# Linear attention and Fourier-mixing MLP: the output products of the chunk pairs regrouped by row mode, under a new order of all engines

## The chip, the cores and the metric

The kernel runs on one core of a Trainium2 chip. The metric is device time in microseconds (us) of one execution. Before the change three runs gave 195.79, 196.08 and 197.27 us, so a median of 196.08 us. The engines are TensorE (PE; its weight loads are PEld), VectorE (DVE), ScalarE (ACT), GpSimd (POOL) and SyncE (SP, which here issues the loads and stores).

## The reference

The inputs are r, k, v, w of shape (4 batches, 8 heads, 768 steps, 48), u of (8, 48), and the weights w_ch1 (384 x 1536) and w_ch2 (1536 x 384). Cut to what matters:

```python
# linear attention with a decaying state, per batch and head
for t in range(S):
    cur = einsum('bhd,bhe->bhde', u * k[t], v[t])
    y[t] = einsum('bhd,bhde->bhe', r[t], state + cur)
    state = w[t][..., None] * state + einsum('bhd,bhe->bhde', k[t], v[t])
# then, with x = y laid out as (4, 768, 384)
mixed = real(fft(fft(x, axis=1), axis=2))
u = x + mixed
un = (u - mean(u)) / sqrt(var(u) + 1e-6)
out = u + maximum(un @ w_ch1, 0) @ w_ch2
```

## The kernel before, in words

**Tiling.** Each batch's 768 steps are cut in six chunks of 128. A chunk's decays become exponentials of running sums (matmuls at L755 and L759, in the first batch L615 and L616), r and k are scaled by them (`rkh`), transposed, and multiplied into a 128 x 128 score block per head (`amat`, L681 or L825), which VectorE masks into `ah` (L687 or L838). The output of a chunk is a masked product of `ah` with v plus r times the state before the chunk.

**The first batch goes in chunk pairs** (`pair`, from L592). Two chunks are loaded interleaved, so that a chunk's rows lie in one half of the 128 partitions, once for even steps and once for odd ones. Its products therefore use 64 of TensorE's 128 rows. In `ymat` (L719 to L731) a chunk's output takes: two half-row matmuls with the bonus term (L721, 384 columns each), and then for each of four head pairs one full-row matmul with the state (L725, 96 columns; not for the first chunk, which has no state yet) and four half-row matmuls with `ah` (L729, 48 columns each). All add up in one PSUM bank. There are six such outputs, five of them with the state. `state` (L701 to L711) is likewise one full-row matmul (L703) and eight half-row ones (L707). The other three batches go chunk by chunk (`attention`), where only `amat` (L825) uses fewer than 128 rows.

**After a batch's attention** its output is folded (`fold`: sums and differences, `xf`), mixed by two rounds of matmuls (L944, L945, L947; then L970), normalised, transposed, and sent through the two MLP products (W1 at L1017, W2 at L1035). W1 and W2 are loaded by one transfer each, issued on GpSimd's queue (L586).

**Order.** The kernel records every operation with the tiles that it reads and writes, and then places them by two tables that were computed in advance: `ORDER` lists each engine's operations by number, `BANKS` lists which PSUM bank holds which tile when. Engines run their list strictly in order and wait on semaphores for what an operation needs from another engine. The times that stand in the `op(...)` calls served the planner that made the tables; they do not enter the emitted program. Where VectorE, ScalarE or GpSimd may do an operation, the table also decides which one does.

**Filler.** `early` issues NE matmuls on a constant tile (L1055) at the start, and NW further operations of the same kind (`warm`, L1072 and L1073) stand in the table between real work. Their results are not used. All operations that only move data through `vec`, `evict` and the like show the helper's line (L450, L473, L474), so they are told apart by their tiles.

Of the kernel before, what the change touches and what calls it, by code (L numbers as in the profile page):

```python
# [20 lines left out]
NE = 13  # L21

NW = 5
# [37 lines left out]
    "act": (  # L61
# [12 lines left out]
    "dve": (  # L74
# [71 lines left out]
class _Prog:  # L146
# [17 lines left out]
    def op(self, eng, dur, fn, r=(), w=(), sem=None, xfer=0, port=(), tiled=False):  # L164


        if not isinstance(dur, dict):
            dur = {eng: dur}
# [156 lines left out]
def bass_rwkv6_finch__then__fnet_fourier_mix_kernel(  # L325
# [11 lines left out]
    DM = H * D  # L337
# [86 lines left out]
    def ps(t):  # L424
        return BANK[t.bank]
# [5 lines left out]
    def mm(n, x=1):  # L431
        return int(x * max(25, n / 2.4 + 2.5))
# [674 lines left out]
```

How the kernel before makes its waits and increments, by code:

```python
        def run(name, eng):  # L271
            for o in self.order[name]:
                for c, v, d in sorted(o.waits, key=lambda x: x[2].at):
                    eng.wait_ge(sems[c], d.val)
                ins = o.fn(eng)
                if o.sem is not None:
                    ins.then_inc(sems[o.sem], 16)
                elif o.inc:
                    ins.then_inc(sems[name], 1)
            if name == "dve":
                for s in dcount:
                    if s.startswith("out"):
                        eng.wait_ge(sems[s], dcount[s])
                eng.nop()
```

## Time and profile before

| | us |
|---|---|
| median of three runs | 196.08 |
| the three runs | 195.79, 196.08, 197.27 |
| the profiled execution | 194.64 |
| its span, first to last instruction | 192.8 |
| TensorE busy | 183.7 (95%) |
| VectorE busy | 154.4 (80%) |
| ScalarE busy | 123.3 (64%) |
| GpSimd busy | 103.2 (54%) |

A TensorE matmul's busy time is longer than the step to the next matmul, because matmuls are pipelined: what one costs is read from the starts of successive rows. PEclk is the clock that TensorE was granted, as a share of full speed; it has two levels, 1.2 and 2.4 GHz. The program is cut below into stretches by start time: the pairs of the first batch run until about 36 us, its mixing until about 50 us, the other batches' attention together with earlier batches' MLP until about 140 us, and the last MLP from there to the end.

### The profile page before, as it was taken

The numbers are of one execution on the slowest core, as the hardware profiler recorded it, in microseconds if no ns is written. First come the engines' busy times: TensorE is split into PE (matmuls) and PEld (weight loads), VectorE is DVE, ScalarE is ACT, GpSimd is POOL, SyncE is SP. The second block draws the span as 40 slices with busy tenths as digits, with TensorE's granted clock in tenths as the row PEclk, the third lists the DMA queues.
The fourth block names the chain that finished last, engine by engine and source line by source line (L and its number), as shares of the span: only waits on it lengthen the run. The fifth ranks groups of instructions, "written<-read, shape, count | busy, mean of one in ns | idle before, by whom it ended". The sixth has DMA issues, their size and how long they took to land.

```text
span 192.8 us, 4713 instructions
## 1 busy us (share of the span) xinstructions
PE 183.7 (95%) x1830; PEld 117.4 (61%) x1830; DVE 154.4 (80%) x336; ACT 123.3 (64%) x287; POOL 103.2 (54%) x118
## 2 busy tenths in 40 slices
PE   6989999999998999999999979999999999999994
PEld 3465665676575666666766655565656556556663
DVE  7499987729999999999999999999987951625434
ACT  4699376439999972968989864899375384131200
POOL 3037947429979770999986779478952000000000
PEclk9999999579999999999999999999999999999999
DMA  6999998998999991984997496798900044300143
GB/s 167 323 325 265 232 191 156 185 219 169 214 196 146 187 195 38 188 182 102 217 255 165 86 183 135 149 182 180 180 25 0 3 102 102 119 7 0 52 178 137
DMA packets 104152, 29.59 MB, mean 153 GB/s; under 512 B 98882, under 2 KB 103619, under 8 KB 104131
## 3 DMA queue, kind: packets, MB, share of 16 engines
q1 hardware_dynamic: 102178, 26.95, 62.9%
q0 software_dynamic: 1952, 2.36, 7.6%
q8 instruction: 14, 0.23, 0.5%
q14 instruction: 8, 0.06, 0.1%
HBM read 24.19 MB, written 4.72 MB: 150 GB/s over the span
## 4 chain that ended last, share of the span: by engine, by line
PE 75%; DVE 16%; ACT 3%; DMA 3%; issue 2%; SPq 1%; DVEq 0%
PE bank L1035 22%; PE bank L1017 19%; PE bank L970 5%; PE bank L947 4%; DVE ah L838 3%; DMA in_v<-in_v_dram 3%; PE bank L1055 2%; PE bank L729 2%; PE bank L825 2%; PE bank L725 2%; PE bank L759 1%; PE bank L755 1%; PE bank L883 1%; DVE xf L450 1%; DVE uf L972 1%
## 5 line engine op out<-in xcount | busy, mean ns | idle before, releaser
L1017 PE MATMUL bank<-unt,w 128*128 128x384 bf16 x288 | 55.9, 326 | 0.0
L1024 ACT ACTIVATE ht<-bank 128x384 bf16<-128x384 f32 x80 | 36.9, 501 | 26.2 <-PE bank L1017 26.1
L1035 PE MATMUL bank<-w,ht 128*128 128x384 bf16 (+2 forms) x300 | 52.2, 320 | 0.1
L1035 PEld LDWEIGHTS bank<-w,ht 128*128 128x128 bf16 x300 | 28.0, 98 | 16.3 <-DVE rkh L793 0.3
L1017 PEld LDWEIGHTS bank<-unt,w 128*128 128x128 bf16 x288 | 26.3, 97 | 15.0
L838 DVE TENSOR_TENSOR ah<-bank,msk 128x512 bf16<-128x512 f32 x36 | 23.2, 677 | 0.4 <-PE bank L825 0.4
L1039 DVE SCALAR_TENSOR_TENSOR osb<-bank,rstd,uf 128x384 f32<-128x384 f32 (+2 forms) x25 | 14.6, 594 | 9.6 <-PE bank L1035 5.2
L473 ACT ACTIVATE rkt<-bank 128x512 bf16<-128x512 bf16 (+1 forms) x26 | 18.1, 706 | 1.7 <-PE bank L665 1.2
L450 POOL TENSOR_TENSOR rkh<-in_k,e 128x384 bf16<-128x384 f32 x18 | 18.3, 1019 | 0.5 <-ACT e L774 0.5
L450 POOL TENSOR_TENSOR vtd<-in_v,dc 128x384 f32<-128x384 f32 x17 | 14.6, 856 | 7.2 <-DVE dc L782 5.7
L450 POOL TENSOR_TENSOR rk<-rk,ub 128x384 f32<-128x384 f32 x17 | 17.3, 1017 | 1.2 <-DVE rk L450 0.8
L1022 DVE TENSOR_SCALAR ht<-bank 128x384 bf16<-128x384 f32 x16 | 8.6, 553 | 11.4 <-PE bank L1017 10.3
L450 POOL TENSOR_TENSOR rk<-in_r,in_k 128x384 f32<-128x384 f32 x16 | 16.6, 1038 | 1.9 <-DMA in_r<-in_r_dram 1.0
L947 PE MATMUL bank<-k,xf 128*128 128x193 bf16 (+1 forms) x84 | 14.4, 280 | 1.9 <-DVE xf L450 1.9
L972 DVE TENSOR_TENSOR uf<-bank,x 128x384 f32<-128x384 f32 x24 | 12.8, 545 | 1.4 <-PE bank L970 1.4
L464 ACT ACTIVATE lb<-in_w 128x384 bf16<-128x384 f32 (+1 forms) x21 | 12.1, 578 | 2.4 <-DMA in_w<-in_w_dram 2.4
L464 ACT ACTIVATE un<-uf,agg 128x384 bf16<-128x384 f32 x21 | 12.2, 629 | 2.0 <-DVE agg L978 2.0
L976 DVE BATCH_NORM_STATS2 bst<-uf 128x6 f32<-128x384 f32 x24 | 12.9, 548 | 0.1
L774 ACT ACTIVATE e<-bank 128x392 f32<-128x392 f32 (+1 forms) x18 | 9.1, 508 | 2.7 <-PE bank L768 2.2
L889 DVE TENSOR_TENSOR x<-bank,vtd 128x384 f32<-128x384 f32 x18 | 9.9, 551 | 1.1 <-PE bank L883 0.9
L464 ACT ACTIVATE vb<-in_v 128x384 bf16<-128x384 f32 (+1 forms) x17 | 10.1, 592 | 0.7 <-DMA in_v<-in_v_dram 0.7
L947 PEld LDWEIGHTS bank<-k,xf 128*128 128x128 bf16 x84 | 7.3, 101 | 5.2 <-DVE xf L450 3.4
(145 smaller groups left out, 369.5 us busy)
## 6 DMA issues: line engine op xcount, KB each, us to landing
out_dram<-osb SPq DMA_DIRECT2D x23, 192.0 KB, 2.1
in_w<-in_w_dram SPq DMA_DIRECT2D x18, 192.0 KB, 4.1
in_v<-in_v_dram SPq DMA_DIRECT2D x18, 192.0 KB, 4.3
in_r<-in_r_dram SPq DMA_DIRECT2D x18, 192.0 KB, 3.8
in_k<-in_k_dram SPq DMA_DIRECT2D x18, 192.0 KB, 3.9
w<-in_moe_w_ch_dram POOLq DMA_DIRECT2D x2, 1152.0 KB, 10.2
in_w<-in_w_dram SPq DMA_DIRECT2D x3, 384.0 KB, 4.0
in_k<-in_k_dram SPq DMA_DIRECT2D x3, 384.0 KB, 4.9
```

Of the source, the lines that this page charges most:

```text
L450: return lambda e: e.tensor_tensor(out=o, in0=a, in1=b, op=f)
L464: return lambda e: e.activation(o, a, f, **kw)
L473: {"act": lambda e: e.activation(o(), i(), ACTF.Copy), "dve": lambda e: e.tensor_copy(out=o(), in_=i())}, **kw)
L838: masked[n] = op("dve", v_1(512), lambda e, x=x: e.tensor_tensor(out=ah[:, x:H:2, :], in0=ps(ta[x])[:, :].rearrange("p (h t) -> p h t", t= ...
L889: op("dve", v_1(DM), lambda e: e.tensor_tensor(out=xb[:, c, 0:DM], in0=ps(ty)[:, 0:DM], in1=vtd[:, :, :].rearrange("t h d -> t (h d)"), op ...
L947: return e.matmul(ps(t)[:, cols], x, tab[:, s % NP, cols], start=a, stop=z, skip_group_check=True)
L972: op("dve", v_1(DM), lambda e, kb=kb, t=t: e.tensor_tensor(out=uf[:, kb, :], in0=ps(t)[:, 0:DM], in1=xb[:, kb, 0:DM], op=ALU.add), r=[t, ( ...
L976: op("dve", v_1(DM), lambda e, kb=kb, bs=bs: e.bn_stats(bs[:, :], uf[:, kb, :]), r=[("UF", i, kb)], w=[("BST", n % 4)])
L1017: ins = e.matmul(ps(t)[:, 0:384], W1[:, m, 128 * j:128 * j + 128], unt[:, :, m, :], start=(m == 0), stop=(m == NM - 1))
L1024: "act": lambda e, j=j, t=t, ht=ht: e.activation(ht[:, j, :], ps(t)[:, 0:384], ACTF.Relu, scale=-1.0)},
L1035: ins = e.matmul(ps(t)[:, 0:hi - lo], ht[:, j, 128 * x:128 * x + 128], W2[:, j, lo:hi], start=(j == 0), stop=(j == NJ - 1))
L1039: op("dve", v_1(hi - lo) + 64, lambda e, kb=kb, t=t, o=o, lo=lo, hi=hi: e.scalar_tensor_tensor(out=o[:, lo:hi], in0=ps(t)[:, 0:hi - lo], s ...
```

## The change

In `ymat` of `pair` the half-row matmuls of a chunk's output now all come first (the two bonus products, then sixteen products with `ah`), and the four full-row products with the state come last. The arithmetic is the same but for the order in which terms are added. NE goes from 13 to 8; NW from 5 operations of two matmuls to 12 of one. The tables `ORDER` and `BANKS` were computed anew, with other planning times for some TensorE operations and with a mark for whether an operation begins or ends in half-row mode. In the new tables some operations also change engine: 22 instead of 16 of the W1 evictions (L1022) and 7 instead of 3 of the normalisations are on VectorE, and two scaled reversals of `hcs` leave GpSimd.

```diff
-NE = 13
+NE = 8
-NW = 5
+NW = 12
...
 ORDER = {
     "pe": (
-        "24 52 53 51 55 56 102 99 45 98 100 103 1383 1384 70 69 72 81 146 147 71 87 116 149 118 78 117 75 119 "
+        "24 1383 1384 52 53 51 55 56 1385 98 99 45 70 100 69 71 72 81 1386 102 1387 103 87 1388 75 78 149 146 117 "
...
-            op("pe", 560, amat, r=kts + rts, w=ta[s], tiled=True)
+            op("pe", 250, amat, r=kts + rts, w=ta[s], tiled=3)
...
-                for q in range(HP):
-                    if back:
-                        e.matmul(ps(ty)[:, 96 * q:96 * q + 96], RT[:, 256 * q + 128 * y:256 * q + 128 * y + 128], s_in[:, q, :], start=False, stop=False,
-                                 skip_group_check=True)
-                    for h in (2 * q, 2 * q + 1):
-                        for s in range(2):
-                            ins = e.matmul(ps(ty)[:, D * h:D * h + D], ah[rows, s, h, :], hid(vb)[rows, h, s, :],
-                                           start=False, stop=s == 1, skip_group_check=True)
+                for h in range(H):
+                    for s in range(2):
+                        ins = e.matmul(ps(ty)[:, D * h:D * h + D], ah[rows, s, h, :], hid(vb)[rows, h, s, :],
+                                       start=False, stop=s == 1 and not back, skip_group_check=True)
+                if back:
+                    for q in range(HP):
+                        ins = e.matmul(ps(ty)[:, 96 * q:96 * q + 96], RT[:, 256 * q + 128 * y:256 * q + 128 * y + 128],
+                                       s_in[:, q, :], start=False, stop=True, skip_group_check=True)
                 return ins
-            op("pe", mm(DM, 2) + mm(D, 16) + (mm(96, 4) if cc else 0), ymat,
+            op("pe", 560 + (260 if cc else 0), ymat,
...
-    op("pe", 1600 + 163 * NE, early, r=["WRM"], w=[tw])
+    op("pe", 400 + 163 * NE, early, r=["WRM"], w=[tw])
...
         def warm(e, tx=tx):
-            e.matmul(ps(tx)[:, 0:384], WRM[:, 0:128], WRM[:, :])
             return e.matmul(ps(tx)[:, 0:384], WRM[:, 0:128], WRM[:, :])
-        op("pe", mm(384, 2), warm, r=["WRM"], w=[tx])
+        op("pe", mm(384), warm, r=["WRM"], w=[tx])
```

The changed file has one line more near its top, so its lines from there on are one higher: L721, L725 and L729 are L722, L730 and L726 in it (the half-row ones now stand ahead of the full-row ones).

**TensorE, the output of the fifth chunk of the first batch.** Before (L721 and L729 are half-row, L725 full-row; `st` is the state, `ht` holds `ah` here):

```order
L759 MATMUL bank<-lb,nle 128x384
L755 MATMUL bank<-lb,msk 128x384
L721 MATMUL bank<-vtd,ht 128x384 x2
L725 MATMUL bank<-st,rkt 128x96
L729 MATMUL bank<-vb,ht 128x48 x4
L725 MATMUL bank<-st,rkt 128x96
L729 MATMUL bank<-vb,ht 128x48 x4
```

and now:

```order
L704 MATMUL bank<-st,idw 128x384
L708 MATMUL bank<-vb,rkh 128x96 x8
L756 MATMUL bank<-lb,msk 128x384 x2
L722 MATMUL bank<-vtd,ht 128x384 x2
L726 MATMUL bank<-vb,ht 128x48 x16
L730 MATMUL bank<-st,rkt 128x96 x4
L722 MATMUL bank<-vtd,ht 128x384 x2
```

The alternation, which before goes on for two more rounds, is gone: one passage from half-row to full-row work is left inside an output.

**TensorE, the start of the program.** Before (L1055 is `early`, L615 the first real work, which needs ScalarE's `lb`):

```order
L1055 MATMUL bank<-ht 128x384 x13
L615 MATMUL bank<-lb,ht 128x384
L616 MATMUL bank<-lb,ht 128x384
L624 MATMUL bank<-pb,idw 128x8
L628 MATMUL bank<-onh,lb 128x2 x8
```

and now:

```order
L1056 MATMUL bank<-ht 128x384 x8
L1073 MATMUL bank<-ht 128x384 x2
L616 MATMUL bank<-lb,ht 128x384
L617 MATMUL bank<-lb,ht 128x384
L625 MATMUL bank<-pb,idw 128x8
```

Ten filler matmuls stand ahead of the first real one, where there were thirteen.

**GpSimd, around the issue of the W1 load.** Before (`xf<-x` are pieces of the fold, L586 is the load of W1, `rk<-in_r,in_k` belongs to the second batch):

```order
L450 TENSOR_TENSOR xf<-x 128x192 x3
L450 TENSOR_TENSOR vtd<-in_v,dcp 128x768
L450 TENSOR_TENSOR xf<-x 128x191 x3
L586 DMA w<-in_moe_w_ch_dram 128x3x1536
L450 TENSOR_TENSOR xf<-x 128x192 x2
L450 TENSOR_TENSOR rk<-in_r,in_k 128x384
```

and now:

```order
L451 TENSOR_TENSOR xf<-x 128x192 x2
L451 TENSOR_TENSOR vtd<-in_v,dcp 128x768
L451 TENSOR_TENSOR xf<-x 128x191 x2
L451 TENSOR_TENSOR xf<-x 128x192 x2
L451 TENSOR_TENSOR rk<-in_r,in_k 128x384
L587 DMA w<-in_moe_w_ch_dram 128x3x1536
```

The W1 load has moved behind the fold pieces of the fourth and fifth chunk and behind the first product of the second batch.

## Rows read from the trace of the kernel before

**Rows 1.** The page, part 2: granted clock in 40 equal slices of the span, in tenths.

```profile
PEclk9999999579999999999999999999999999999999
```

**Rows 2.** Busy us by stretch: length, each engine (instructions), granted clock, DMA share, GB/s.

```profile
10.00:25.00 15.00, 13.48 (x226) 9.13 (x222) 14.62 (x24) 11.26 (x18) 9.57 (x7) 1.00 1.03 261
25.00:34.40 9.40, 9.38 (x133) 5.62 (x130) 6.96 (x15) 6.96 (x17) 5.76 (x8) 1.00 0.94 178
34.40:41.30 6.90, 6.90 (x44) 4.52 (x44) 3.39 (x8) 1.30 (x4) 2.57 (x3) 0.51 1.08 204
...
50.00:140.00 90.00, 87.25 (x948) 57.12 (x947) 88.55 (x183) 71.97 (x176) 71.66 (x76) 1.00 0.85 167
...
145.00:190.40 45.40, 45.34 (x297) 28.01 (x294) 23.36 (x51) 14.85 (x37) 1.75 (x2) 1.00 0.21 66
```

**Rows 3.** Timeline of TensorE: start us, us, line, tiles, count [idle before].

```profile
28.86 0.49 PE L721 MATMUL bank<-vtd,ht 64*128 64x384 bf16 x2
29.29 0.22 PE L725 MATMUL bank<-st,rkt 128*128 128x96 bf16 x1
29.43 0.27 PE L729 MATMUL bank<-vb,ht 64*128 64x48 bf16 x4
29.63 0.22 PE L725 MATMUL bank<-st,rkt 128*128 128x96 bf16 x1
...
30.68 0.34 PE L703 MATMUL bank<-st,idw 128*128 128x384 bf16 x1
...
31.40 0.34 PE L759 MATMUL bank<-lb,nle 128*128 128x384 bf16 x1
31.57 0.33 PE L755 MATMUL bank<-lb,msk 128*128 128x384 bf16 x1
31.83 0.49 PE L721 MATMUL bank<-vtd,ht 64*128 64x384 bf16 x2
```

**Rows 4.** Timeline of TensorE: an output without the state, then full-row neighbours later.

```profile
20.85 0.56 PE L729 MATMUL bank<-vb,ht 64*128 64x48 bf16 x16
21.34 0.62 PE L665 MATMUL bank<-idw,rkh 128*128 128x128 bf16 x8
...
56.26 0.21 PE L880 MATMUL bank<-st,rkt 128*128 128x96 bf16 x1
56.30 0.21 PE L883 MATMUL bank<-vb,ah 128*128 128x48 bf16 x2
```

**Rows 5.** Timeline of VectorE in the first batch's mixing.

```profile
42.26 0.60 DVE L474 CAST hcs<-bank 128x386 bf16<-128x386 f32 x1 [3.89 <-PE bank L945]
```

**Rows 6.** Timeline of all engines in the opening.

```profile
1.49 4.34 PE L1055 MATMUL bank<-ht 128*128 128x384 bf16 x13 [1.49 <-DVE ht L461]
...
4.14 0.84 ACT L464 ACTIVATE lb<-in_w 128x768 bf16<-128x768 f32 x1 [2.14 <-DMA in_w<-in_w_dram]
...
5.63 0.53 PE L615 MATMUL bank<-lb,ht 128*128 128x384 bf16 x1
```

**Rows 7.** Timeline of GpSimd around the two weight loads.

```profile
31.54 0.97 POOL L586 DMA_DIRECT2D w<-in_moe_w_ch_dram  x1
36.27 1.62 POOL L450 TENSOR_TENSOR xf<-x 128x192 bf16<-128x192 f32 x2 [3.76 <-ACT x L473]
37.85 0.99 POOL L450 TENSOR_TENSOR rk<-in_r,in_k 128x384 f32<-128x384 f32 x1
...
57.95 1.10 POOL L586 DMA_DIRECT2D w<-in_moe_w_ch_dram  x1
```

**Rows 8.** Line L586, the two weight loads: us from issue to landing.

```profile
DMA to landing us min/median/max: 9.5/10.2/10.9
```

**Rows 9.** Timeline of TensorE: first use of W1 and of W2.

```profile
49.64 2.11 PE L1017 MATMUL bank<-unt,w 128*128 128x384 bf16 x12
...
69.57 2.11 PE L1035 MATMUL bank<-w,ht 128*128 128x384 bf16 x12
```

**Rows 10.** Groups by line: W1 evictions on VectorE, busy us, mean ns, idle before.

```profile
L1022 DVE TENSOR_SCALAR ht<-bank 128x384 bf16<-128x384 f32 x16 | 8.6, 553 | 11.4 <-PE bank L1017 10.3 <-PE bank L1035 1.1
```

More of the change, by code:

```diff
@@ L162, in tile, with op @@
         return t
-    def op(self, eng, dur, fn, r=(), w=(), sem=None, xfer=0, port=(), tiled=False):
+    def op(self, eng, dur, fn, r=(), w=(), sem=None, xfer=0, port=(), tiled=0):
         if not isinstance(dur, dict):
@@ L539, in bonus @@
         t = g.tile("f")
-        op("pe", mm(384, 4), lambda e: e.matmul(ps(t)[:, 0:DM], ONF[0:1, :], UR[0:1, :]), r=["ONF", "UR"], w=[t])
+        op("pe", 420, lambda e: e.matmul(ps(t)[:, 0:DM], ONF[0:1, :], UR[0:1, :]), r=["ONF", "UR"], w=[t])
         o = evict(lambda: UB[:, :, :].rearrange("p h d -> p (h d)"), lambda: ps(t)[:, 0:DM], DM, r=[t, "LOGEXP"], w=["UB"])
@@ L564, in rows @@
                 return ins
-            op("pe", 100 + mm(HE, len(moves[j])), rows, r=["IDB", "NIDW"] + ["CS", "SS"], w=[t])
+            op("pe", (165, 450, 180)[j], rows, r=["IDB", "NIDW"] + ["CS", "SS"], w=[t])
             evict(lambda j=j: DTM[:, j, 0:HE], lambda t=t: ps(t)[:, 0:HE], HE, r=[t], w=["DTM%d" % j])
@@ L711, in state @@
                     return ins
-                op("pe", mm(96, 8) + (mm(DM) if cc else 0), state, r=[("KH", i) for i in i4] + [("VB", i) for i in i4]
-                   + ([("ST", (cc + 1) % 2), "IDB"] if cc else []), w=[tds])
+                op("pe", 350 + (260 if cc else 0), state, r=[("KH", i) for i in i4] + [("VB", i) for i in i4]
+                   + ([("ST", (cc + 1) % 2), "IDB"] if cc else []), w=[tds], tiled=2 if cc else 3)
                 op("dve", v_1(DM), lambda e, tds=tds, we=we, s_out=s_out: e.tensor_tensor(
@@ L722, in ymat @@
                              hid(vtd)[rows, :, s, :], start=s == 0, stop=False, skip_group_check=True)
-                for q in range(HP):
-                    if back:
-                        e.matmul(ps(ty)[:, 96 * q:96 * q + 96], RT[:, 256 * q + 128 * y:256 * q + 128 * y + 128], s_in[:, q, :], start=False, stop=False,
-                                 skip_group_check=True)
-                    for h in (2 * q, 2 * q + 1):
-                        for s in range(2):
-                            ins = e.matmul(ps(ty)[:, D * h:D * h + D], ah[rows, s, h, :], hid(vb)[rows, h, s, :],
-                                           start=False, stop=s == 1, skip_group_check=True)
+                for h in range(H):
[6 more added lines that the diff above has]
+                                       s_in[:, q, :], start=False, stop=True, skip_group_check=True)
                 return ins
-            op("pe", mm(DM, 2) + mm(D, 16) + (mm(96, 4) if cc else 0), ymat,
+            op("pe", 560 + (260 if cc else 0), ymat,
                r=[("AHP", h2, s, x) for s in range(2) for x in range(2)] + [("VB", i) for i in i4] + [("VTD", i4[0]), "PRM"]
-               + (rts + [("ST", (cc + 1) % 2)] if cc else []), w=[ty])
+               + (rts + [("ST", (cc + 1) % 2)] if cc else []), w=[ty], tiled=1 if cc else 3)
             evict(lambda cc=cc: X[b % 2][:, cc, 0:DM], lambda ty=ty: ps(ty)[:, 0:DM], DM, r=[ty], w=[("X", b % 2, cc)])
@@ L827, in amat @@
             return ins
-        op("pe", 207, amat, r=[("KTB", i4), ("RTB", i4)], w=ta, tiled=True)
+        op("pe", 207, amat, r=[("KTB", i4), ("RTB", i4)], w=ta, tiled=3)
         for x in range(2):
```

147 rows, old and new, of tables (BANKS, ORDER) are left out of this document.

## The prediction

> **What bounds the kernel now.** I read the page's busy times first, then the busy time by stretch, and then timelines. TensorE is busy 183.7 of 192.8 us, VectorE 154.4 (the table of the section on time and profile). By stretch [rows 2] TensorE is nearly full from 25 us on (9.38 of 9.40, then 6.90 of 6.90, 87.25 of 90.00, and 45.34 of 45.40 at the end), and VectorE is nearly full too from 10 to 25 us (14.62 of 15.00) and from 50 to 140 us (88.55 of 90.00). So the time is TensorE's list plus its few waits, with VectorE close behind. A busy TensorE is not one that streams columns all the time, and two things inside its busy time can be taken out.
>
> The first is the granted clock. It stands at the lower level, 1.2 GHz, for the whole stretch from 34.4 to 41.3 us [rows 1, 2]. VectorE is busy for only 3.39 us of these 6.90, and at 42.26 it has stood idle for 3.89 us until TensorE's L945 [rows 5].
>
> The second is the alternation in the pair outputs. Two full-row matmuls of 384 columns start 0.17 us apart (31.40 to 31.57); when the next one is half-row the same step is 0.26 (31.57 to 31.83) [rows 3]. A full-row one of 96 columns takes 0.14 to 0.15 when half-row ones follow (29.29 to 29.43) [rows 3], and 0.04 among full-row neighbours (56.26 to 56.30) [rows 4]. Four half-row ones of 48 columns take 0.20 until the next full-row one (29.43 to 29.63) [rows 3]; sixteen in a row take 0.49 until a full-row one (20.85 to 21.34) [rows 4], so less one passage about 0.39, or 0.10 for four. Each passage between the modes thus costs about 0.10 us, in either direction.
>
> **The change part by part**, against the profiled execution's 194.64 us, which stands 1.44 under the median of 196.08.
>
> *Regrouped outputs.* An output with the state took 1.82 us (28.86 to 30.68) [rows 3]. Now it is 2 x 0.17 + 0.39 + one passage 0.10 + 4 x 0.04 = 0.99, so 0.83 less where full-row work follows and 0.73 where half-row work does. Per output seven passages go; five outputs have the state, so 35. Counted over the whole orders, passages go from 96 to 58: three more went by placing half-row operations side by side. 38 x 0.10 = 3.8 us. One of the five outputs lies before 25 us, where VectorE leaves only 0.38 us of 15; I count its 0.7 us as hidden, which leaves **-3.1** (bounds -3.8, and -2.0 if a third of the rest becomes waiting).
>
> *The low clock.* What TensorE did ahead of the fall was exactly these outputs: 1.82 us for 2 x 384 + 16 x 48 + 4 x 96 = 1920 columns, which is 0.80 us of streaming at 2.4 GHz, 44% of the time, and most of it on half the rows; regrouped, the same 0.80 us lie in 0.99. If the sparse stretch is what let the clock fall, it now stays up, and 6.9 us at half rate become 3.4: **-3.4** (bounds 0 and -3.4). What would be late next is the chain from the last output over its eviction and fold into the mixing; in the old kernel that chain had the low-clock stretch as cover, since TensorE was busy all through it.
>
> *Filler.* Ten filler matmuls instead of thirteen stand ahead of L615. Thirteen took 1.49 to 5.63, 0.32 each, so three are 0.96; but ScalarE's `lb` is done at 4.14 + 0.84 = 4.98, so the gain is at most 0.65 [rows 6]. What follows waits for loads and ScalarE as well: **-0.3** (bounds 0 and -0.65). Of later filler there were five pairs, and there are ten single ones (two of the twelve stand in the opening, counted above): the same number at 0.17 each [rows 3], so **0** (bounds 0 and 0.5, if they now fall into denser work).
>
> *The weight loads.* W1 was issued at 31.54 [rows 7]; a landing takes 9.5 to 10.9 us [rows 8]; so it was there at 41.0 to 42.4, and first used at 49.64 [rows 9], 7 us later. Now it stands on GpSimd behind fold pieces of the fourth and fifth chunk and one product. The old piece at 36.27 waited 3.76 us for the last chunk's eviction [rows 7]; the fifth chunk's is one output, 1.8 us, earlier: 34.5, less 3.1 gained is 31.4, plus one piece (1.62 / 2 = 0.8) and the product (0.99) is 33.2. W1 lands at 42.7 to 44.1, and TensorE now wants it at 49.64 - 6.8 = 42.8. So the wait is 0 to 1.3, and all of TensorE's list queues behind it: **+0.3**. W2 landed at latest at 57.95 + 10.9 = 68.9, just ahead of 69.57 [rows 7 to 9]; its first use is now at about 63.1, so it must be issued by 52.2. Two reversals of `hcs` have left GpSimd ahead of it and the waits on the slow mixing go, so I take 0 (bounds 0 and the rival below).
>
> *Changed engines.* Six more W1 evictions on VectorE are 6 x 0.55 = 3.3 us [rows 10], but most stand behind the attention in VectorE's list, where VectorE is busy 23.36 of 45.40 us [rows 2]: 0, covered by the last MLP's matmuls. In the middle stretch they would cost their full price.
>
> *TensorE's waits.* The new order has other waits. In rows 2 they are 1.52 us (10 to 25) and 2.75 (50 to 140); I take them unchanged (bounds: a third gone, or half as much again, -1.4 to +2.1).
>
> Sum: -3.1 - 3.4 - 0.3 + 0.3 = -6.5, so 188.1 for an execution like the profiled one and **189.6** for the median of runs.
>
> **The rivals.**
>
> *The clock falls all the same*: 193.0 (189.6 + 3.4). For it: the sparse part has not gone everywhere, the pair stretch still holds transposes, scores and states in short matmuls, and five filler matmuls fewer stand at the start, so the clock may also rise later. Against: the fall came behind the last outputs of the batch, and the alternation in them is gone. A rule points this way: the Trainium skill (TensorE: Matmul & The Clock Gate, section Why this matters for your kernels) ties a mid-kernel drop to idle gaps between bursts of matmuls, and by it sparse but gapless outputs would not matter and their regrouping would not hold the clock. The trace does not agree so far: TensorE was busy 9.38 of the 9.40 us ahead of the fall [rows 2]. Chance 17%.
>
> *VectorE becomes the bound*: 191 to 193, say 192. From 25 to 41.3 us VectorE is idle for 2.44 + 3.51 = 5.95 us [rows 2], and about 6 us are to be cut from there, so it would have to run without a gap. If it reaches 90% there, its 10.35 us of work take 11.5 instead of 10.1: +1.4, and the evictions placed early some more. Against: ScalarE and GpSimd have room. Chance 13%.
>
> *The change does not do what it says*: the steps of 0.14 to 0.15 belong to something else than the mode, say the state's arrival, and only the clock is gained: 196.08 - 3.4 = 192.7. Against: the same 0.10 shows at L755 to L721, where no state is read [rows 3]. Chance 4%.
>
> *Slower: a late W2 holds TensorE, and the clock falls behind that idle time.* The place is the first L1035, the price 68.9 - 63.1 = 5.8 us if GpSimd reaches W2 no earlier than before, with W1's wait at its upper end 1.0 more, and another low stretch of 3.4: 189.6 + 10.2 = 199.8. It decides from an issue of W2 after 52.2; with the clock still up the result is no change, 196.4. For it: W2 had under 1 us to spare, and both loads stand in a list that runs strictly in order. Against: what delayed GpSimd was the slow mixing, which shrinks. Chance 9%.
>
> **How the numbers follow.** The forecast has 57%, its own range 187.5 to 191.5 from the bounds above. The range 186.5 to 194.0 takes in the clock and VectorE rivals, and at its lower end the waits that a new order can remove; it leaves out the slower case and a few of the others. About 1% (194.1 to 198.0) is what three runs that spread by 0.8% can tell from no change. Faster by more: the forecast and most of the next three, 82%; within 1%: 9%; slower: 9%.
>
> **What would show it.** In the changed profile: L730's four matmuls at steps of 0.04 and an output in about 1.0 us; PEclk at 9 from its rise to the end; the mixing of the first batch (L971) beginning 6 to 7 us earlier; L587's landings ahead of the first L1018 and L1036. It is wrong if a low stretch stands anywhere behind the opening, if TensorE's first L1018 or L1036 shows a wait, or if VectorE is full from 25 us on with TensorE waiting for it.

## The result

The changed kernel takes 188.55 us, the median of four executions (187.31, 189.78, 190.04, 186.52), where the kernel before took 196.18 in four beside it. The ratio is 0.9519, 95% interval 0.9446 to 0.9593: it is faster, by 4.8%. The forecast of 189.6 is 1.05 us above that. The ratio leaves out executions over 1.5% above a kernel's fastest; since the clock that TensorE is granted differs between executions of one and the same kernel, the medians of all executions and the mean granted clock of each are given with it below.

### The profile page after: what moved, and what is told of

The parts are those of the page before. It is cut to its first block, busy times and chain, and to the rows that moved or that the text cites. A ratio compares the mean times of both kernels' runs of the same rounds, so it can differ in the third digit from the quotient of the medians.

```text
span 185.5 us, 4700 instructions
## 1 busy us (share of the span) xinstructions
PE 176.3 (95%) x1827; PEld 115.0 (62%) x1827; DVE 155.8 (84%) x346; ACT 119.3 (64%) x280; POOL 100.0 (54%) x115
## 4 chain that ended last, share of the span: by engine, by line
PE 70%; DVE 18%; DMA 6%; ACT 3%; issue 1%; SPq 0%; ACTq 0%
PE bank L1036 22%; PE bank L1018 19%; PE bank L971 5%; PE bank L948 5%; DVE ah L839 3%; DVE bst L977 2%; DMA unt<-un 2%; DMA in_v<-in_v_dram 2%; PE bank L826 2%; DMA in_w<-in_w_dram 2%; DVE uf L973 2%; PE bank L726 1%; PE bank L722 1%; DVE rkh L794 1%; PE bank L760 1%
## 5 line engine op out<-in xcount | busy, mean ns | idle before, releaser
L1018 PE MATMUL bank<-unt,w 128*128 128x384 bf16 x288 | 55.5, 326 | 0.6 <-DMA unt<-un 0.5
L1036 PE MATMUL bank<-w,ht 128*128 128x384 bf16 (+2 forms) x300 | 53.3, 320 | 0.0
L1025 ACT ACTIVATE ht<-bank 128x384 bf16<-128x384 f32 x74 | 34.4, 496 | 28.3 <-PE bank L1018 28.1
L1036 PEld LDWEIGHTS bank<-w,ht 128*128 128x128 bf16 x300 | 27.8, 98 | 15.9
L1018 PEld LDWEIGHTS bank<-unt,w 128*128 128x128 bf16 x288 | 26.3, 97 | 16.2 <-DMA unt<-un 0.9
L451 POOL TENSOR_TENSOR rkh<-in_k,e 128x384 bf16<-128x384 f32 x20 | 20.6, 1028 | 9.9 <-ACT e L634 8.4
L1023 DVE TENSOR_SCALAR ht<-bank 128x384 bf16<-128x384 f32 x22 | 11.6, 547 | 5.5 <-PE bank L1036 5.1
L948 PE MATMUL bank<-k,xf 128*128 128x193 bf16 (+1 forms) x84 | 11.6, 258 | 0.0
L465 ACT ACTIVATE un<-uf,agg 128x384 bf16<-128x384 f32 x17 | 10.4, 627 | 0.1
L465 ACT ACTIVATE vb<-in_v 128x384 bf16<-128x384 f32 (+1 forms) x17 | 9.4, 558 | 1.6 <-DMA in_v<-in_v_dram 1.6
L794 DVE TENSOR_TENSOR rkh<-bank,in_r 128x384 bf16<-128x384 f32 x18 | 9.7, 546 | 0.4 <-ACT bank L762 0.4
L762 ACT ACTIVATE bank<-bank 128x384 f32<-128x384 f32 x18 | 8.7, 487 | 2.0 <-PE bank L756 2.0
```

The costliest lines, as they stand in the source:

```text
L451: return lambda e: e.tensor_tensor(out=o, in0=a, in1=b, op=f)
L465: return lambda e: e.activation(o, a, f, **kw)
L948: return e.matmul(ps(t)[:, cols], x, tab[:, s % NP, cols], start=a, stop=z, skip_group_check=True)
L1018: ins = e.matmul(ps(t)[:, 0:384], W1[:, m, 128 * j:128 * j + 128], unt[:, :, m, :], start=(m == 0), stop=(m == NM - 1))
L1023: {"dve": lambda e, j=j, t=t, ht=ht: e.tensor_scalar(out=ht[:, j, :], in0=ps(t)[:, 0:384], scalar1=-1.0, scalar2=0.0, op0=ALU.mult, op1=AL ...
L1025: "act": lambda e, j=j, t=t, ht=ht: e.activation(ht[:, j, :], ps(t)[:, 0:384], ACTF.Relu, scale=-1.0)},
```

## The profile after

The profiled execution is the one of 187.31 us; its span is 185.5 us where it was 192.8. TensorE is busy 176.3 us (183.7 before), VectorE 155.8, ScalarE 119.3, GpSimd 100.0. So all of the 7.3 us came out of TensorE's busy time; its idle time is 9.2 us, where it was 9.1.

The granted clock in 40 slices of the span, from the page after:

```profile
PEclk9998799999999999999999999999999999999999
```

The low stretch of [rows 1] is gone from its place, but the line isn't at 9 throughout: there is another, shorter one much earlier.

The busy time by stretch of the changed kernel; the columns are those of [rows 2]:

```profile
10.00:25.00 15.00, 12.87 (x214) 8.78 (x212) 14.27 (x23) 11.20 (x21) 11.22 (x10) 0.89 1.05 270
15.00:17.00 2.00, 0.52 (x12) 0.35 (x9) 2.00 (x2) 0.54 (x2) 1.37 (x1) 1.00 1.11 389
17.10:20.50 3.40, 3.36 (x32) 1.98 (x30) 3.27 (x6) 2.81 (x4) 2.68 (x2) 0.50 0.78 165
20.50:34.40 13.90, 13.90 (x263) 10.07 (x261) 11.71 (x22) 11.22 (x26) 10.57 (x14) 1.00 0.96 195
34.40:41.30 6.90, 6.90 (x79) 5.21 (x77) 6.59 (x18) 5.35 (x14) 5.00 (x7) 1.00 1.04 191
50.00:140.00 90.00, 88.10 (x963) 59.16 (x961) 86.64 (x182) 70.44 (x175) 66.57 (x71) 1.00 0.85 164
```

From 34.4 to 41.3 us the clock is at its upper level, 2.4 GHz, and 79 matmuls run where 44 ran. From 17.1 to 20.5 it is at the lower one, 1.2 GHz, right behind two microseconds in which TensorE was busy for 0.52 only (it had also waited 0.60 us ahead of L616, until 13.88). What it waited for there is in the timeline (start us, us, engine, line, operation, tiles, count, and in brackets the idle time before it):

```profile
12.48 2.12 POOL L451 TENSOR_TENSOR vtd<-in_v,dcp 128x768 bf16<-128x768 f32 x1 [0.27 <-DVE dcp L644]
...
14.56 1.80 POOL L451 TENSOR_TENSOR uf<-uf,ub 128x768 f32<-128x768 f32 x1
14.72 2.07 DVE L451 TENSOR_TENSOR rkh<-in_k,e 128x384 bf16<-128x384 f32 x1
...
16.84 0.42 PE L666 MATMUL bank<-idw,rkh 128*128 128x128 bf16 x4 [1.48 <-DVE rkh L451]
```

VectorE's product `rkh` begins 0.16 us behind a product on GpSimd and takes 2.07 us. The same form of product on VectorE takes 0.54 at 35.07 in this kernel. TensorE's transposes of the third chunk pair (L666) wait 1.48 us for it.

TensorE's longest waits, L666's among them (engine and line, what it waited for, us in total, times, longest):

```profile
PE bank L1056 <- DVE ht L462: 1.7, 1, 1.7
PE bank L666 <- DVE rkh L451: 1.5, 1, 1.5
PE bank L826 <- DVE rkt L475: 1.2, 1, 1.2
PE bank L616 <- DVE st L715: 0.6, 1, 0.6
PE bank L1018 <- DMA unt<-un: 0.5, 1, 0.5
```

None of them is for a weight load. An output with the state, and the start of the program, on TensorE's timeline:

```profile
5.15 0.50 PE L616 MATMUL bank<-lb,ht 128*128 128x384 bf16 x1
...
25.91 0.49 PE L722 MATMUL bank<-vtd,ht 64*128 64x384 bf16 x2
26.24 0.56 PE L726 MATMUL bank<-vb,ht 64*128 64x48 bf16 x16
26.74 0.34 PE L730 MATMUL bank<-st,rkt 128*128 128x96 bf16 x4
27.01 0.42 PE L682 MATMUL bank<-rkt 48*64 48x128 bf16 x16
...
36.89 0.32 PE L971 MATMUL bank<-k,hcs 128*128 128x384 bf16 x1
...
45.39 0.81 PE L1018 MATMUL bank<-unt,w 128*128 128x384 bf16 x4
...
65.12 0.81 PE L1036 MATMUL bank<-w,ht 128*128 128x384 bf16 x4
```

The output takes 25.91 to 27.01, so 1.10 us, where it took 1.82 [rows 3]. The weight loads, on GpSimd's timeline, and how long they took to land:

```profile
33.88 0.98 POOL L587 DMA_DIRECT2D w<-in_moe_w_ch_dram  x1
...
52.72 1.08 POOL L587 DMA_DIRECT2D w<-in_moe_w_ch_dram  x1
```

```profile
DMA to landing us min/median/max: 10.3/10.8/11.4
```

The first of the two loads, W1, is the one that took 10.3 us: it was there at 44.2, 1.2 us ahead of its first use at 45.39. W2 took 11.4 and was there at 64.1, 1 us ahead of 65.12.

## The experiments

The theory after the result: the regrouped outputs save TensorE's time as forecast, and the clock falls for either of two reasons, the alternation by itself or idle time ahead of it (L666's wait). Its rivals are that idle time alone does it, so that the regrouping has no part in it, and that the new order is what made the kernel faster. Each experiment was run six or more times beside the kernel before on the same chip; the number behind a stroke is the mean granted clock of an execution.

### The changed kernel again (e1)

No edit. Expected:

> The changed kernel as it is, beside the next three on the same chip, to have its spread and the granted clock of each run. Theory 'clock varies': its runs fall in groups by granted clock, one lower stretch of 3.4 us at about 186.5 to 187.5 and longer ones at about 190. Rival 'one clock': all runs within 0.5 us, and the 186.5 to 190.0 seen so far came from elsewhere.

Measured: 190.48 us median, 190.94/0.973, 189.99/0.973, 187.12/0.991, 191.30/0.973, 191.09/0.973, 190.02/0.973; the kernel before 197.32. L666's wait of 1.5 us is there again, and the clock falls behind it again, but for longer:

```profile
17.60:27.90 10.30, 10.30 (x113) 6.71 (x111) 8.46 (x14) 5.77 (x12) 7.33 (x7) 0.50 0.95 193
```

So 6.9 us more at the lower level, and the execution (190.94) is 3.6 us longer than the one of 187.31: in this stretch the low clock costs about half of its length. The kernel doesn't reach a granted clock of 1.00 in any of ten executions.

### The alternation back, in the new order (e2)

```diff
-                for h in range(H):
-                    for s in range(2):
-                        ...
-                if back:
-                    for q in range(HP):
-                        ...
+                for q in range(HP):
+                    if back:
+                        e.matmul(... RT ...)
+                    for h in (2 * q, 2 * q + 1):
+                        for s in range(2):
+                            ...
```

> The changed kernel, its new order and filler kept, but each pair output alternates again between one full-row and four half-row matmuls. Theory 'passages': 35 passages of 0.10 us come back, and all but the ones of the output before 25 us cost time: +2.8 to +3.5 us against the changed kernel with the clock unchanged, and up to 3.4 more if the sparse outputs let the clock fall. Rival 'the new order did it': the alternation is hidden behind VectorE and the difference stays under 1 us.

Measured: 196.65 us median (195.09 to 198.33), clock 0.938 to 0.956; the ratio to before is 1.0159 (1.0012 to 1.0306). The ratio sets e2 at clock 0.956 against before at 0.982. At 0.956 in both, e2's four executions average 196.0 us and the eight of before 197.2: the new order alone gains about 1 us. The profile (196.25) has the fall at 17.7 us, as in e1, and a second one from 38.1 to 45.0, which e1 has not: 17.1 us at the lower level in all.

```profile
PEclk9998569958999999999999999999999999999999
```

Ahead of the second fall TensorE had no idle time at all:

```profile
28.70:38.10 9.40, 9.40 (x139) 5.75 (x135) 5.37 (x11) 6.74 (x14) 3.67 (x5) 1.00 0.99 193
38.10:45.00 6.90, 6.90 (x47) 4.77 (x47) 2.30 (x6) 1.60 (x5) 2.47 (x3) 0.51 1.09 199
```

The medians of e2 and e1 are 6.2 us apart, the two profiled executions 5.3. Of these, 3.4 are half of the 6.8 us more of low clock, and 1.9 are left for the 35 passages; of TensorE's busy time, which is 6.3 us longer (185.5 against 179.2), 2.9 are.

### VectorE's late product moved to GpSimd (e3)

The one `rkh` product of 2.07 us stands on GpSimd, ahead of the product that it collided with (operation 115 ahead of 108 in the table).

```diff
-        "82 62 107 88 112 80 115 114 76 ...     (dve)
+        "82 62 107 88 112 80 114 76 ...
-        "... 32 28 63 108 153 ...               (pool)
+        "... 32 28 63 115 108 153 ...
```

> The changed kernel, with one product moved: the scaled k of the fourth chunk (rkh<-in_k,e), which took 2.07 us on VectorE at 14.72 while GpSimd ran its own product of 1.80 us from 14.56, and for which TensorE waited 1.48 us at 16.84, is now done on GpSimd ahead of that product. Theory 'port': VectorE's product waited for GpSimd's, so on GpSimd it takes 1.0 us from 14.6, TensorE's wait shrinks by about 1.2 us, and if the low clock behind it came from that idle time the stretch at 17 us goes too (1.7 more): -1.2 to -2.9 us. Rival 'GpSimd late': GpSimd's later products move back by 1.0 us and TensorE waits for the bonus terms of the second pair instead: 0 or slower.

Measured: 189.82 us median: 190.67/0.982, 185.12/1.00, 184.49/1.00, 189.06/0.982, 190.57/0.982, and one execution of 607.07 that nothing explains. L666 now waits 0.21 us, and nothing falls at 17 us in the profile (190.67). But the clock falls at 44.7, behind waits for another engine, which begin on SyncE (SPq is the engine's issue of a transfer):

```profile
33.65 4.62 SPq L500 DMA_DIRECT2D in_r<-in_r_dram  x1
38.31 3.08 SPq L500 DMA_DIRECT2D in_k<-in_k_dram  x1
```

```profile
41.69 0.99 POOL L451 TENSOR_TENSOR rk<-in_r,in_k 128x384 f32<-128x384 f32 x1 [4.20 <-DMA in_k<-in_k_dram]
```

The issue at 33.65 stands 1.5 us behind that of W1 (32.18) and lasts 4.62 us; `in_k` behind it comes late, GpSimd waits for it, and TensorE for GpSimd's `rkh` (L816, 3.8 us in two waits). From 40.0 to 44.6 TensorE was busy 2.11 us of 4.60. Take one idle time away, and in this execution the clock falls behind the next. The two executions of 184.49 and 185.12, at clock 1.00, are the fastest of all kernels here.

### The wait filled (e4, and e12 on a third chip)

Nine filler matmuls stand directly ahead of L666's waiting transposes. The wait stays; TensorE isn't idle in it.

```diff
-                def tr(e, x=..., t=t, i=i):
+                def tr(e, x=..., t=t, i=i, fill=9 * (c == 2 and i == 0 and nm == "RH")):
+                    for _ in range(fill):
+                        e.matmul(ps(t)[:, 0:384], WRM[:, 0:128], WRM[:, :])
```

> The changed kernel, with nine more filler matmuls of 384 columns (1.5 us at 0.16) issued just ahead of TensorE's 1.48 us wait at 15 us, so that TensorE waits as long but streams. Theory 'idle time let the clock fall': granted clock 1.00 from its rise to the end in the profile, -1.7 us in a run with one low stretch. Rival 'the sparse pair work lets it fall wherever it is': a low stretch stays, at 17 us or elsewhere, and the time is the same or up to 0.3 us longer.

> The kernel of e4 once more, as the base for e9 and e10 on the same chip: 186.0 to 187.0, granted clock 1.00 throughout.

Measured: e4 186.53 us median (186.00 to 188.01), e12 186.35 (186.09 to 187.08). The granted clock is 0.999 or 1.00 in all twelve executions, and from the opening to the end in the profile. On e1's chip it is 3.95 us faster than the changed kernel, and the spread has shrunk to 2 us. Ratios to before: 0.9680 (0.9602 to 0.9757) and 0.9649 (0.9597 to 0.9702). It is the best steady version.

```profile
14.89 1.62 PE L666 MATMUL bank<-ht 128*128 128x384 bf16 x9
16.35 0.81 PE L668 MATMUL bank<-idw,rkh 128*128 128x128 bf16 x8
```

### The regrouping alone, in the old order (e5)

The kernel before, with `ymat` as in the change's diff and nothing else.

> The kernel before with its own order, banks and filler; only the pair outputs are regrouped (half-row matmuls first). Theory 'passages, then the clock': 35 passages of 0.10 us go (-2.8 to -3.5) and the outputs ahead of the fall at 34.4 us are denser, so the low stretches shrink too, by 3.4 to 5.1 us: about -6 to -8 us, near the changed kernel. Rival 'the new order is needed': the old order leaves the freed time as waits on VectorE: less than -2 us.

Measured: 194.57 us median: 195.46/0.974, 189.30/1.00, 189.46/1.00, 194.94/0.973, 195.26/0.982, 194.19/0.981; ratio 0.9842 (0.9707 to 0.9976). In the profile (195.46) TensorE's saved time turns into waits:

```profile
PE bank L970 <- POOL hcr L961: 4.0, 1, 4.0
PE bank L815 <- POOL rkh L450: 1.7, 1, 1.7
...
PE bank L1035 <- DMA w<-in_moe_w_ch_dram: 1.3, 1, 1.3
```

The clock falls at 40.1, in the idle time ahead of L970 (busy 1.78 us of 4.10 from 36.0 to 40.1), and W2 is late, as the slower rival had it.

### Filler in the old outputs (e6)

The kernel before, alternation and all, with three filler matmuls ahead of each of four outputs, so that TensorE streams more without a change of order.

```diff
-            def ymat(e, rows=rows, s_in=s_in, ty=ty, back=cc > 0, y=y):
+            def ymat(e, rows=rows, s_in=s_in, ty=ty, back=cc > 0, y=y, fill=3 * (cc > 1)):
+                for _ in range(fill):
+                    e.matmul(ps(ty)[:, 0:DM], WRM[:, 0:128], WRM[:, :])
```

> The kernel before, alternation and all, with three filler matmuls of 384 columns ahead of each of the last four pair outputs: 12 x 0.16 = 1.9 us more work for TensorE, no wait and no passage removed. Theory 'sparse streaming lets the clock fall, not idle time': the granted clock holds from its rise to the end or nearly so, and a run at 0.956 (17 us at half rate, so 8.5 us lost) becomes one 8.5 - 1.9 = 6.6 us shorter; one low stretch of 6.8 us still left would make that 3.2. Rival 'only idle time counts': TensorE had none there, so the clock falls as before and the time is 1.9 us longer.

Measured: 195.05 us median: 197.01/0.983, 195.95/0.991, 193.53/0.991, 195.24/0.991, 194.87/0.991, 194.24/1.00. The clock is up from 0.956, which most executions before have, but the filler costs what it gives back: at full clock 194.24 stands against 190.82 for before on this chip. And it doesn't hold the clock: in the profile (197.01) it falls at 36.8, with TensorE busy 9.39 of the 9.40 us ahead. So more streaming inside the outputs made the low stretches fewer or shorter, while e4, without the alternation, has none; whether it is the few columns or the passages themselves that let the clock fall, these runs do not separate.

### More filler at the start, clock held (e7)

```diff
-NE = 8
+NE = 13
```

on top of e4.

> The changed kernel with the filled wait of the run before (nine filler matmuls at 15 us) and thirteen instead of eight matmuls at the start. Theory 'opening': five more at the lower level are 1.6 us, of which 0.3 to 0.4 is TensorE's wait for ScalarE's first lb; the rest delays the start of the real work: +0.3 to +1.2 us against the filled kernel. Rival 'earlier rise': the denser opening lets the clock rise sooner and the time is the same or up to 0.5 shorter.

Measured: 188.90 us median (187.51 to 189.12), clock 1.00 in all six; 2.4 us more than e4, which ran on another chip (e12, on a third, is 0.2 from e4). The first real matmul starts at 6.42 instead of 5.14, which is 1.28 of it; the rest are TensorE's waits for transfers (W2 0.4, `rkt` 0.9 instead of 0.3, `unt` 0.6 instead of 0.1).

### W1 one place later, on top of e3 (e8)

```diff
-        "... 138 178 376 198 207 405 "    (pool)
+        "... 138 178 376 207 198 405 "
```

> The kernel with rkh of the fourth chunk on GpSimd, and the issue of the W1 load moved one place later on GpSimd, behind its first copy of hcr for which it waits 1.9 us anyway. In that kernel's profile a load issued just behind W1 was held up for 4.6 us on SyncE's queue, the next in_k behind it came late, GpSimd waited 4.2 us for it and TensorE 3.8 us in all at 42 to 46 us, where the clock then fell. Theory 'W1 crowds out in_k': with W1 2 to 3 us later the two loads go first, TensorE's wait there shrinks to under 1 us and the clock holds in most runs: about 184.5 to 185.5. Rival 'W1 late': TensorE waits for W1 at the first L1018 by 1 to 3 us: 186 to 188.

Measured: 186.91 us median (185.74 to 189.73), clock 0.991 or more; ratio 0.9684 (0.9591 to 0.9778). `in_k` is on time, but W1, issued at 34.57, isn't:

```profile
45.08 3.30 PE L1018 MATMUL bank<-unt,w 128*128 128x384 bf16 x12 [1.82 <-DMA w<-in_moe_w_ch_dram]
```

The clock falls at 45.9, behind this idle time: TensorE was busy 3.26 of the 5.90 us from 40.0 to 45.9. This kernel is ready for L1018 at 43.26 and waits for W1 until 45.08; the changed kernel, with W1 issued at 33.88, gets to L1018 at 45.39 only, 1.2 us after W1 has landed.

### The wait filled and the alternation back (e9)

Both edits, e2's and e4's.

> The changed kernel with its 15 us wait filled (as e4) and with the old alternation back in the pair outputs; the order is unchanged. Theory 'the alternation lets the clock fall by itself, with no idle time before it': 35 passages come back, 0.10 each, of which 2 to 3.5 us reach the end, and a low stretch of 3.4 to 10 us stands in the pair outputs (1.7 to 5 us): 190.5 to 195. Rival 'only idle time lets it fall': clock 1.00 to the end, and the price is that of the passages alone, 188.5 to 190.

Measured: 194.54 us median (188.92 to 199.14, 14 executions), clock 0.939 to 1.00; ratio 0.9952 (0.9789 to 1.0114). Two executions have 1.00: 188.92 and 189.55. The profile (196.43/0.956):

```profile
14.50:23.10 8.60, 8.33 (x125) 5.27 (x124) 7.90 (x12) 4.91 (x10) 5.50 (x5) 1.00 1.00 255
19.00:23.10 4.10, 4.02 (x79) 2.67 (x79) 3.40 (x7) 2.27 (x6) 2.23 (x3) 1.00 0.95 208
23.10:26.60 3.50, 3.50 (x31) 2.58 (x28) 3.46 (x6) 2.34 (x6) 3.50 (x5) 0.51 0.89 173
```

With L666's wait filled the clock still falls, at 23.1, and TensorE had been busy 4.02 of the last 4.10 us; its work there begins with an output with alternation, 19.10 to 20.91. That is the fall of the kernel before [rows 2], without idle time. The clock is back at 26.6 and falls once more at 30.0, now for 13.7 us, with TensorE busy 10.00 of the 10.00 us ahead:

```profile
20.00:30.00 10.00, 10.00 (x151) 6.94 (x150) 6.88 (x12) 5.43 (x12) 5.19 (x7) 0.83 1.02 210
30.00:43.65 13.65, 13.65 (x113) 7.54 (x113) 6.51 (x15) 6.08 (x15) 6.11 (x8) 0.50 1.01 194
```

All profiled falls behind the opening part in the same way. Those without idle time ahead (before, the second of e2, e6, both of e9, e11) are all in kernels with the alternation; every fall of a regrouped kernel (after, e1, e3, e5, e8), and e2's first, stands behind idle time, with TensorE busy for 1.6 to 2.1 of the 4 us ahead.

### VectorE's copy of `rkt` earlier, on top of e4 (e10)

```diff
-        "449 423 507 452 475 476 ...      (dve)
+        "507 449 423 452 475 476 ...
```

> As e4 (wait filled), and VectorE's copy of rkt at 55 us, for which TensorE's L828 waits 1.2 us, stands three places earlier in VectorE's list. Theory 'TensorE's waits reach the end one for one from 25 us on': the wait falls to 0 to 0.3, time 185.4 to 185.9 where e4 has 186.5. Rival 'the state's product that is now behind the copy (L870) holds the next full-row products, and the time comes back': 186.3 to 186.8.

Measured: 186.57 us median (186.19 to 187.78), e12 beside it 186.35: no change. Both theories missed why:

```profile
PE bank L828 <- DVE x L892: 1.2, 1, 1.2
```

The score product L828 waits for two things, the copy of `rkt` and the bank that `x` is read from (L892); the profile had named the one that came last. With the copy out of the way the wait is as long as before, for the other. The edit moves the copy two places, not three, and it made the other later itself: the copy now stands ahead of that `x` in VectorE's list, and `x` begins at 55.49 where it began at 54.89 in e4, while the `x` before it moved by 0.27 only (52.11, 51.84).

### The short opening alone (e11)

The kernel before with NE = 8.

> The kernel before with 8 instead of 13 filler matmuls at the start, nothing else. Forecast's term: the first real matmul starts at about 5.0 instead of 5.63, and 0.3 of that reaches the end: 195.8 where before has 196.1. Theory from e7 (five filler matmuls more cost 2.4 us in the changed kernel): 1.3 to 2.4 us less, 193.7 to 194.8. Rival: the clock rises later or falls earlier without the filler, 196 or more.

Measured: 194.07 us median (189.99 to 198.53, 12 executions), before 196.39; ratio 0.9919 (0.9805 to 1.0033), so not told apart from no change. Where the clock was 1.00 it is 189.99, and before 189.79 and 190.17. What it may gain is clock (0.982 in eight of twelve executions, where before has mostly 0.956), not work: L615 starts at 5.40 instead of 5.63 (forecast 5.0), behind a wait of 1.16 us for `lb`.

## Why the prediction was right

The result lies inside the range, 1.05 us under the forecast; the regrouping did what it was said to do. The clock did not: the prediction calls itself wrong "if a low stretch stands anywhere behind the opening", and one does. That the total came out all the same is in part luck, as the terms show. The executions at full clock, from all the runs, tell the work apart from the clock:

| kernel, executions at clock 0.999 or 1.00 | us |
|---|---|
| before (3) | 189.79, 190.17, 190.82 |
| e5, regrouped in the old order (2) | 189.30, 189.46 |
| e9, new order with alternation, wait filled (2) | 188.92, 189.55 |
| e4 and e12, new order regrouped, wait filled (12) | 186.00 to 188.01, median 186.46 |

And how many executions hold the clock:

| | L666's wait left | wait filled |
|---|---|---|
| alternation, new order | e2: none of 6 | e9: 2 of 14 |
| regrouped, new order | after and e1: none of 10 | e4, e7, e10 and e12: 24 of 24 |

*Regrouped outputs, -3.1: right.* An output ahead of half-row work now takes 1.10 us, 0.72 less (the forecast had 0.73), and the four L730 with the passage behind them 0.27 (4 x 0.04 + 0.10). Between e9 and e12 at full clock the regrouping is worth 2.6 to 3.2 us. In the old order it is worth 0.9 to 1.4 only (e5's two against the mean of the three of before, or against the one on its own chip, 190.82). The waits shown there took its place in the profiled execution; at full clock no profile of e5 shows it. So the forecast's bound for lost cover, -2.0, was not low enough for that order, and it is the new order that lets the rest through.

*Low clock, -3.4: the cause was half the cause, and the size came out by other numbers.* That the alternation lets the clock fall with TensorE busy is shown (e9, and the fall in [rows 2]). That the clock would then stay up to the end is the step that failed: the sentence "If the sparse stretch is what let the clock fall, it now stays up" took it for the only cause. Behind L666's wait of 1.5 us it fell again, earlier, for 3.4 us in the profiled execution and 10.3 in e1; only with both causes gone does it hold (24 of 24). In the profiled executions the gain is half of 6.8 - 3.4, so -1.7. In the medians it is larger, since most executions of before lose more than the profiled one: 196.08 less the mean at full clock, 190.26, is 5.8 us; the changed kernel loses 188.55 less about 185.6 (187.31 less half of its 3.4 us), so 2.9. The difference is -2.9; with e4's and e12's 186.46 for the changed kernel at full clock, it is -3.7. So the size of the forecast's -3.4 came about because both kernels mostly lose more than their profiled executions show, and not by a clock that stayed up: that is luck.

*The rival of the clock that falls all the same, 193.0,* thus came true in part, and was weighed on the wrong evidence: the rows ahead of the old fall spoke against idle time as its cause there, not against idle time as a cause elsewhere. The rule of the Trainium skill (TensorE: Matmul & The Clock Gate, section Why this matters for your kernels) warns of idle gaps between bursts of matmuls that are longer than the one here. The trace agrees with it in kind only: the changed kernel's clock fell behind 1.48 us of idle time, and e4 held it by filling that. The rule doesn't cover the falls of before and of e9, where TensorE was busy 9.38 of 9.40 us and 4.02 of 4.10 us.

*TensorE's waits, unchanged: right in sum, and where one stands mattered more than the sum.* From 10 to 25 us they went from 1.52 to 15.00 - 12.87 = 2.13 us, from 50 to 140 from 2.75 to 1.90. The forecast priced a new wait at its length. L666's costs 1.4 to 2.0 us (e3's two at full clock against e4's median on the same chip) and, where it isn't filled, 1.7 to 5 us of clock behind it.

*New order, 0: about -1.* With the alternation back it is 188.92 and 189.55 at full clock, before 189.79 and 190.17 on the same chip, so -0.7, from two executions each; e2 at clock 0.956 gives -1.2.

*Filler, -0.3: not settled.* L616 starts at 5.15, 0.48 earlier than L615 did. The short opening alone gives between -3.8 and +0.6 (e11's interval), nothing at full clock; five more filler matmuls with the clock held cost 2.4 (e7), but they begin the work later than before's opening did.

*Weight loads, +0.3: 0.* W1 was issued at 33.88 (forecast 33.2), landed at 44.2 and was used at 45.39, not at 42.8: the mixing began at 36.89 instead of 42.62, 5.7 us earlier, but L1018 only 49.64 - 45.39 = 4.25 earlier [rows 9]. With the issue one place later, on top of e3, TensorE waits 1.82 for it (e8). W2 was issued at 52.72, 0.5 behind the forecast's limit, and L1036 came 4.45 us earlier, not 6.5, so the slower rival did not come about; in the old order the same regrouping made W2 late (e5).

*Changed engines, 0: no cost shown.* From 50 to 140 us VectorE is busy 86.64 us where it was 88.55.

*VectorE as the bound: no.* From 20.5 to 34.4 us it is busy 11.71 of 13.90 with TensorE at 13.90. But its one late product opens the way for the clock's fall.

The sum of TensorE's busy time: 38 passages 3.8, low clock 1.7, three filler matmuls 1.0, so 6.5 of the 7.4 us that went; the other 0.9 stays open. Also open: why the same fall lasts 3.4 us in one execution and 10.3 in another, what else differs between executions of the same mean clock (e11's eight at 0.982 take 191.61 to 195.28), and the one of 607 us.

## What to carry to other kernels

TensorE's granted clock had two causes of falling here, gapless outputs that alternate between half-row and full-row matmuls and a short idle time, and taking away one only moves the fall: look, for each fall, at the busy time ahead of it, and price a new wait of TensorE with the clock behind it. Where executions of one kernel differ, compare those at full granted clock, where the work stands apart from the clock; an equal mean clock below 1.00 is not enough. Time saved on the fullest engine reaches the end only as far as the order lets the next engine keep up: at full clock the same edit was worth 0.9 to 1.4 us in the old order and about 2.9 in the new one.

## What the hardware showed that was not expected

VectorE's 384-wide product of two SBUF tiles took 2.07 us when it began 0.16 us behind a 768-wide product on GpSimd (14.56 to 16.36), and 0.54 to 0.56 where none ran beside it; 14.72 to 16.36 is 1.64, and 1.64 + 0.54 = 2.18 is about what it took, so it seems to have stood until GpSimd was done. In e1 it is 2.07 again, and on GpSimd itself the product takes 1.00 (e3). The Trainium skill (SBUF — State Buffer, section Who interferes with whom) states a lock that VectorE, with two SBUF inputs, and GpSimd hold in turn for a whole instruction; the trace agrees with it, 2.07 against 0.54 us. The kernel before shows both orders: at 22.48, inside a product on GpSimd (21.87 to 23.69), VectorE's takes 1.63; at 15.26, begun 0.16 us ahead of one, it takes 0.55 and GpSimd's takes 2.06 instead of 1.80 to 1.82.

An issue of a load on SyncE that begins some 2 us behind that of a weight load on GpSimd takes far longer than its neighbours: 5.64 us at 36.39 in the changed kernel (W1 at 33.88; 0.66 to 2.55 for those around it), 4.62 in e3, where TensorE's late `rkh` came from it. It is so in all fourteen traces, for W1 and for W2: an issue that begins 1.3 to 3.5 us behind takes 4.0 to 6.2 us, but for W1 in e8, where the long one, 4.16, begins 6.3 us behind. The issues ahead of the long one, behind the weight load's, take at most 2.0 us (3.2 in e8). What holds it the runs do not show.

```profile
35.64 0.71 SPq L500 DMA_DIRECT2D in_r<-in_r_dram  x1
36.39 5.64 SPq L500 DMA_DIRECT2D in_w<-in_w_dram  x1
42.08 2.55 SPq L500 DMA_DIRECT2D in_v<-in_v_dram  x1
```
